# Blocks of 32x32 and VectorE's transpose in place of TensorE's, for the third and fourth quarter of a gated attention

## What is computed

```
state = alpha[t][:, None] * state + outer(k[t], v[t])
y[t]  = q[t] @ state
```

## Time and profile before

| | |
|---|---|
| median of three runs | 690.23 us |
| span of the profiled execution, first to last instruction | 689.6 us |
| TensorE busy | 680.8 us, 99% |
| VectorE busy | 461.4 us, 67% |
| GpSimd busy | 327.2 us, 47% |
| ScalarE busy | 266.4 us, 39% |
| TensorE clock granted | 1.00 all through |

### The profile page before, as it was taken

One profiled execution on the slowest core, in us unless ns is written; L12 is line 12 of the kernel. 1 busy time (PEld: TensorE's weight loads), 2 busy tenths in 40 slices (PEclk: granted clock), 3 DMA queues, 4 the chain that ended last, 5 costly groups with the idle time before them and its releaser, 6 DMA issues.

```text
span 689.6 us, 10745 instructions
## 1 busy us (share of the span) xinstructions
PE 680.8 (99%) x3987; PEld 632.7 (92%) x3987; DVE 461.4 (67%) x820; ACT 266.4 (39%) x485; POOL 327.2 (47%) x416
## 2 busy tenths in 40 slices
PE   8999999999999999999999999999999999999998
PEld 7788999999999999998999999999999999999997
DVE  6875747555565544118978867886787678767876
ACT  4524533223522252227534333433343334343430
POOL 3569561111111116773394567456745674577200
PEclk9999999999999999999999999999999999999999
DMA  9896490009102001000011110111011101100003
GB/s 154 163 217 173 106 139 1 10 2 118 20 5 74 1 1 47 1 5 19 1 47 46 47 47 0 47 47 46 1 47 48 46 1 47 46 24 1 23 1 138
DMA packets 72230, 34.56 MB, mean 50 GB/s; under 512 B 53872, under 2 KB 71664, under 8 KB 72176
## 3 DMA queue, kind: packets, MB, share of 16 engines
q1 hardware_dynamic: 71728, 33.85, 22.8%
q10 hardware_dynamic: 448, 0.00, 0.0%
HBM read 30.89 MB, written 2.36 MB: 48 GB/s over the span
## 4 chain that ended last, share of the span: by engine, by line
PE 92%; SPq 3%; DVE 1%; POOL 1%; DMA 1%; issue 1%; ACT 0%; POOLq 0%
PE out_ps L1453 13%; PE out_ps L1454 13%; PE out_ps L1455 13%; PE hid_ps L1446 7%; PE hid_ps L1448 7%; PE hid_ps L1447 6%; PE at_ps L1708 5%; PE at_ps L1707 5%; PE at_ps L1706 4%; PE hid_ps L1707 2%; PE hid_ps L1708 2%; PE hid_ps L1706 2%; SPq L488 2%; PE at_ps L1531 2%; PE at_ps L1545 1%; PE at_ps L1585 1%
## 5 line engine op out<-in xcount | busy, mean ns | idle before, releaser
L1329 DVE SCALAR_TENSOR_TENSOR x<-out_ps,prob,x 128x384 f32<-128x384 f32 x180 | 110.3, 613 | 57.8 <-PE out_ps L1455 57.8
L1454 PE MATMUL out_ps<-early_r,late_r 128*128 128x384 f32 x384 | 129.4, 337 | 0.0
L1455 PE MATMUL out_ps<-early_r,late_r 128*128 128x384 f32 x384 | 129.3, 337 | 0.0
L1453 PE MATMUL out_ps<-early_r,late_r 128*128 128x384 f32 x384 | 129.0, 336 | 0.0
L722 POOL TENSOR_TENSOR hid_lo<-act_sb,hid_hi 128x384 fp32r<-128x384 f32 x44 | 44.8, 1019 | 159.6 <-ACT hid_hi L949 159.6
L999 ACT COPY late<-at_ps 128x512 f32<-128x512 f32 x105 | 61.8, 588 | 101.8 <-PE at_ps L1708 98.7
L1295 DVE TENSOR_TENSOR act_sb<-hid_ps,act_sb 128x384 f32<-128x384 f32 x48 | 26.0, 541 | 79.1 <-PE hid_ps L1448 79.1
L1453 PEld LDWEIGHTS out_ps<-early_r,late_r 128*128 128x128 f32 x384 | 72.1, 188 | 6.1 <-DVE x L1329 0.2
L1454 PEld LDWEIGHTS out_ps<-early_r,late_r 128*128 128x128 f32 x384 | 72.0, 188 | 5.6
L1455 PEld LDWEIGHTS out_ps<-early_r,late_r 128*128 128x128 f32 x384 | 72.1, 188 | 0.0
L949 ACT CAST hid_hi<-act_sb 128x384 fp32r<-128x384 f32 x48 | 24.6, 512 | 83.9 <-DVE act_sb L1295 83.9
(11 more groups left out here) (301 smaller groups left out, 1617.4 us busy)
## 6 DMA issues: line engine op xcount, KB each, us to landing
stage<-in_moe_w_dram SPq DMA_DIRECT2D x32, 384.0 KB, 3.6
stage<-in_moe_w_out_dram SPq DMA_DIRECT2D x4, 576.0 KB, 5.4
out_dram<-x SPq DMA_DIRECT2D x12, 192.0 KB, 1.9
stage<-in_moe_w_gate_dram SPq DMA_DIRECT2D x8, 216.0 KB, 4.1
stage<-in_moe_w_val_dram SPq DMA_DIRECT2D x8, 216.0 KB, 4.2
a_tm<-in_alpha_dram SPq DMA_DIRECT2D x9, 192.0 KB, 4.5
k_tm<-in_k_dram SPq DMA_DIRECT2D x9, 192.0 KB, 5.4
q_tm<-in_q_dram SPq DMA_DIRECT2D x9, 192.0 KB, 5.3
```

The lines of the kernel that those rows point to most:

```text
L1329: dve.scalar_tensor_tensor(out=a, in0=part, scalar=p, in1=a, op0=ALU.mult, op1=ALU.add).then_inc(s_acc, 1)
L1453: pe.matmul(dst, ah, bh, start=first, stop=False)
L1454: pe.matmul(dst, ah, bl, start=False, stop=False)
L1455: return pe.matmul(dst, al, bh, start=False, stop=last)
```

## The change

For the third and fourth quarter (`i >= BY_DVE`, 2) the loads place alpha, keys and queries as blocks of 32 tokens by 32 columns, so that VectorE's transpose, which turns each 32x32 block by itself, gives the same layout that TensorE's transposes gave. A DMA fills 32 partitions with 12 blocks; a pair takes four DMAs, a quarter 16 for each of the three tensors in place of 3. Rows behind the 48 columns of a head then hold the first values of the next token in place of ones; the products mask them. VectorE transposes 128x384 elements at once into the same PSUM banks: alpha in step T, keys and queries in step KQ ahead of the two multiplications. TensorE's steps T, TQ and AHEAD of these quarters go.

```diff
+        SQ = 32
+        NSQ = TQ // SQ
+        LANES = P // SQ
+        BY_DVE = 2
+        def squares_of(t, n):
+            return t[:, :, :].rearrange("p c x -> p (c x)")[:, n * TQ:(n + 1) * TQ]
+        def rows_arrived(i):
+            return 16 * (NCH * min(i + 1, BY_DVE) + LANES * NP * max(i + 1 - BY_DVE, 0))
...
-                        if 3 * f + sub == 3 * (FT - 2) + 2 and i + 2 < NQ:
-                            yield "AHEAD", i + 2, 0
...
+            def load_squares(i, which):
+                b, t0 = i // QB, (i % QB) * TQ
+                src, dst, done = ((alpha, a_tm, s_qka[0]), (k, k_tm, s_qka[1]), (q, q_tm, s_qka[2]))[which]
+                for n in PAIR_ORDER:
+                    home = squares_of(dst, n).rearrange("p (j x) -> p j x", x=SQ)
+                    for lane in range(LANES):
+                        first = lane % 2 * SQ
...
+                        rows = bass.AP(src.tensor, src.offset + ((b * H + 2 * n + lane // 2) * S + t0) * D + first,
+                                       [[D, SQ], [SQ * D, NSQ], [1, width]])
+                        sp.dma_start(home[lane * SQ:(lane + 1) * SQ, :, 0:width], rows).then_inc(done, 16)
...
-                load_quarter(i, 0)
+                (load_squares if i >= BY_DVE else load_quarter)(i, 0)
...
-                    load_quarter(i, which)
+                    (load_squares if i >= BY_DVE else load_quarter)(i, which)
...
+                if i >= BY_DVE:
+                    dve.wait_ge(s_qka[1], rows_arrived(i))
+                    dve.transpose(banks[2][:, :], squares_of(k_tm, PAIR_ORDER[f])).then_inc(s_tk, 1)
+                    dve.wait_ge(s_qka[2], rows_arrived(i))
+                    wait_three(dve, s_yc, i, f, 2)
+                    dve.transpose(banks[0][:, :], squares_of(q_tm, PAIR_ORDER[f])).then_inc(s_tq, 1)
                 own_done()
                 dve.wait_ge(s_tk, u + 1)
...
-                        dve.wait_ge(s_qka[0], 16 * NCH * (i + 1))
+                        dve.wait_ge(s_qka[0], rows_arrived(i))
...
+                    if i >= BY_DVE:
+                        dve.wait_ge(s_clamp, i + 2)
+                        dve.transpose(banks[1][:, :], squares_of(a_tm, PAIR_ORDER[f])).then_inc(s_ta, 1)
                     dve.wait_ge(s_ta, u + 1)
...
-                if name in ("T", "TQ") and i >= 2 and f == 0:
+                if name in ("T", "TQ") and i >= BY_DVE:
                     continue
...
                     pe.wait_ge(s_qkd, 2 * u + 1)
+                    if i >= BY_DVE:
+                        wait_three(pe, s_yc, i, f, 2)
```

More of the change, by code:

```diff
@@ L490, in load_quarter @@
                                  ).then_inc(arrived or done, 16)
+            def load_squares(i, which):
[5 more added lines that the diff above has]
+                        first = lane % 2 * SQ
+                        last = (b, t0, n, lane) == (B - 1, S - TQ, NP - 1, LANES - 1)
+                        width = D - SQ if last else SQ
+                        rows = bass.AP(src.tensor, src.offset + ((b * H + 2 * n + lane // 2) * S + t0) * D + first,
+                                       [[D, SQ], [SQ * D, NSQ], [1, width]])
+                        sp.dma_start(home[lane * SQ:(lane + 1) * SQ, :, 0:width], rows).then_inc(done, 16)
             def fill_holes(i):
@@ L1141, in _ @@
                 elif name == "T":
+                    dec, k_dm, q_dm, _, _, banks, _ = own_of(i, f)
+                    if i >= BY_DVE:
+                        dve.wait_ge(s_clamp, i + 2)
+                        dve.transpose(banks[1][:, :], squares_of(a_tm, PAIR_ORDER[f])).then_inc(s_ta, 1)
                     dve.wait_ge(s_ta, u + 1)
@@ L1144, in _ @@
                         dve.wait_ge(s_st, NCH * NP)
-                    dec, k_dm, q_dm, _, _, banks, _ = own_of(i, f)
                     for c in range(NCH):
@@ L1502, in _ @@
                     name = "Y"
-                if name in ("T", "TK", "TQ", "AHEAD", "S", "KV", "Y", "AV"):
+                if name in ("T", "TK", "TQ", "S", "KV", "Y", "AV"):
                     n = PAIR_ORDER[f]
                     _, k_dm, q_dm, k_sm, sc_sb, banks, y_bank = own_of(i, f)
-                if name in ("T", "TK", "TQ", "AHEAD"):
-                    todo = {"AHEAD": ((0, a_tm, 1, s_ta), (1, k_tm, 2, s_tk), (2, q_tm, 0, s_tq)),
-                            "T": ((0, a_tm, 1, s_ta), (1, k_tm, 2, s_tk))[:2 if i else 1],
+                if name in ("T", "TK", "TQ"):
+                    todo = {"T": ((0, a_tm, 1, s_ta), (1, k_tm, 2, s_tk))[:2 if i else 1],
                             "TK": ((1, k_tm, 2, s_tk),), "TQ": ((2, q_tm, 0, s_tq),)}[name]
```

## The result

The changed kernel takes 683.58 us in the median of four runs (683.46 to 684.27), the kernel before 690.45 in four. The ratio is 0.9897 with a 95% interval of 0.9885 to 0.9909, so the change saves 7.1 us, 6.3 to 7.9. The forecast was 682.7 us. The kernel is faster, as forecast; its median is 0.9 us above the forecast one.

A forecast was written before the change was run, and what follows sets the result against it. TensorE, busy 680.8 of 689.6 us, was taken as the bound, with VectorE's transposes and the loads hidden: 689.6 - 7.6 = 682.0 us of span, plus 0.6 around it, gave 682.7 us; range 681 to 688.

The forecast's parts named there:

- TensorE's removed transposes: 72 transposes leave TensorE: six pairs by 0.98 us, quarter ends 0.70 and 0.99, 7.6 us saved in all.
- The hole at the rounding: At the second quarter's end the last O product waits for ScalarE's rounding, about 0.3 us; 0.70 saved, not 0.99.
- Spare at the first pair: VectorE's scaled queries against the scores: a transpose may take 0.82 us; at 0.55, 0.8 us is left.
- The rival of the reciprocal's pace: VectorE becomes the bound: a transpose takes 2.55 us, scaled queries come late, kernel 722.4 us; chance 0.05.
- the one of the scan's pace: VectorE's transpose takes 1.05 us, like three scans; 3.8 us lost, still faster at 686.5 us; chance 0.08.
- that of 0.93 us: Three VectorE transposes at the skill's 311 ns make 0.93 us, past the 0.82 and 0.92 allowed: 683.5 us; no chance given.
- The loads: 48 DMAs a quarter on one queue, 0.5 us an issue: hidden, 1.5 us to spare for alpha, 8 for queries.
- the rate of pieces: Block loads: about 849 pieces per us, so a DMA's 384 take 0.45 us; supports 0.5 us between issues.
- The deadline of 120.6 us: Third quarter: the queries' transpose must begin by 120.6 us, so an issue may take 0.66 us.
- the slow rivals: VectorE becomes the bound, 722.4 us, chance 0.05; block loads arrive late, 705.4 us, chance 0.08.
- No gain: TensorE waits in every column for V product, multiplication, rounding as long as it had transposed: 690 us; chance 0.05.
- The 0.6 us around the span: Time outside the profiled span, taken as before: 0.6 us added to 682.0 us of span gives 682.7 us.

The follow-up runs named there:

- v_first: Changed kernel with VectorE multiplying V's sums before normalising the next block's input at the second quarter's end; one run, 684.5 us.
- the kernel with the transposes in place: Kernel before, with first pairs' TensorE transposes in T and TQ instead of AHEAD: old loads 691.69 us, ratio 1.0012; block loads 691.01 us, ratio 1.0003.
- loads_only: Changed kernel's block loads alone, TensorE transposing as before with AHEAD and VectorE transposing nothing: 696.32 against 691.02 us for the kernel before, ratio 1.0077.

## Why the prediction was right

- TensorE's removed transposes. Forecast 7.57 us, found 7.24 by distance and 7.1 by time. The working by starts held to 0.08 us at every place. It promised too much at the pairs of the third quarter, where V's first matmuls now come straight behind the output matmuls of 48 columns: V's product takes 128.65 - 126.96 = 1.69 us, and took 130.51 - 128.87 = 1.64. At the end of the second quarter the second matmul behind the stand came 0.1 us later than worked out; it had stood 0.26 us behind the first before the change too, and the working put it at 0.17.
- The hole at the rounding. Forecast 0.3 us, found 0.28; v_first shows that the rounding made it.
- VectorE. Taken 0.55 us for a transpose, found 0.55 to 0.59. Spare at the first pair 0.8 forecast, 0.92 found. Doubling the transposes cost 4.8 us by distance where the same chain gave 5.5. The chain was read from the third quarter alone: there a pair cost 0.65 to 0.69, near the 0.6 expected, and in the fourth only 0.22 to 0.26, since its queries end at 202.18 + 0.54 = 202.72 against scores at 204.43, 1.7 us to spare. TensorE's waits in these runs stand at the transposes of the scaled keys, a place that the forecast passed over; it lost nothing by that, as the queries are the tighter ones. The rival of the reciprocal's pace, the one of the scan's pace and that of 0.93 us are out by the rows of the transpose. The Trainium skill (VectorE: DVE Perf Modes, "The three transpose paths") has 311 ns for 128x128 in bf16; the trace has 0.55 to 0.59 us for 128x384 in float32, so its figure is no price for each block of 128 columns.
- The loads. The queries landed at 112.8 us as forecast, nearly 6 us before they were wanted, but that the number fits is luck: 0.50 us was taken between issues and 0.51 to 0.58 found, which makes 48 issues 2.5 us longer, and 5.3 us was taken from issue to landing and 2.3 found, 3.0 shorter; the first issue came 0.5 us later. The margin did not hang on either. The reason given for 0.50, the rate of pieces, did not hold: an issue costs nearly that with half the pieces too. The rule on transfers under 512 bytes (the Trainium skill, DMA: Bandwidth & Descriptors, "Specifications") had no price here: with pieces of 128 bytes in place of 192 the kernel with the transposes in place kept every distance. Two things were missing in that step. The deadline of 120.6 us holds only because AHEAD goes, which was not said; loads_only shows it with 5.3 us. And a late load costs more than its lateness, since the clock falls: the slow rivals would probably have been dearer than they were priced.
- No gain. TensorE stands for the chain V product, multiplication, rounding only once, at the end of the second quarter, as worked out; this rival is out.

The mechanism is right and the sum nearly so, but part of its nearness is luck. TensorE's working promised 0.3 us too much. The 0.6 us around the span was mis-sized: it set the span of one execution against the times of others, while a run's own time lies 1.7 to 1.9 us above its own span in both kernels (683.49 and 681.8 after, 690.65 and 688.8 before), some 1.2 us more. Against these two the start of the profiled execution after came 0.68 us earlier, which nothing in the change explains. Together they leave about the 0.9 us between forecast and median.

## What to carry to other kernels

Where one engine fills the span, work taken from it is gained place by place, and what it is worth is read from starts, not from durations. The engine that takes the work over needs slack in the chain up to the next handover; its share of idle time says little, and the slack can be read from the end of that chain and the start of who waits for it. When an early step is removed or kept, look at the deadline that it sets for the loads: here its removal made many small DMAs free, and the same loads with the old step cost 5 us.

## What was not expected of the hardware

- The cost of a stand of TensorE. After 3.3 us of standing the granted clock fell to 0.50, which cost 1.7 us more. With stands of 2 us at eight pairs the kernel lost 29 us where they add up to 16; the clock fell behind seven of them and not behind the fifth, of the same length, so a short stand's price is not the same each time.
- The pace of SyncE's DMA issues. 0.48 to 0.53 us with 192 pieces of 128 bytes and 0.51 to 0.58 with 384, both into 32 partitions: half the pieces save 0.05 us of 0.55. A DMA of 48 KB landed 2.3 us after its issue, one of 192 KB 5.3 us before the change.
- The transposes of VectorE, 128x384 float32 from SBUF into PSUM: 0.55 to 0.59 us, about the same as a multiplication of that size (0.54). The forecast had taken 0.55, but no row before the change showed it.
